# An attention scan and two expert layers on one core: the first chunk's scores in one readout, its y without a state, k turned on TensorE

## What is computed

```python
for t in range(S):                                   # S = 768, state 48 x 48 per head
    cur = einsum('bhd,bhe->bhde', u * kt, vt)
    y[:, :, t] = einsum('bhd,bhde->bhe', rt, state + cur)
    state = wt[..., None] * state + einsum('bhd,bhe->bhde', kt, vt)
x = y as 3072 tokens x 384
h = maximum(maximum(x @ w1, x @ w2), x @ w3); x = h @ w_out            # 384 -> 768 -> 384
h = x @ w_in; solu = h * softmax(h); out = layernorm(solu, g) @ w_out2  # 384 -> 1024 -> 384
```

## Time and profile before

| | us |
|---|---|
| median of 3 runs (lowest, highest) | 797.6 (792.9, 798.09) |
| the profiled execution | 798.28 |
| its span, first to last instruction | 796.4 |
| PE busy in the span | 744.8 (94%) |
| DVE busy | 502.3 (63%) |
| ACT busy | 296.6 (37%) |
| POOL busy | 70.6 (9%) |

### The profile page before, as it was taken

How to read it: one execution, slowest core, us unless ns; L and a number is a source line. 1 busy time by engine, 2 the same in 40 slices (tenths; PEclk the granted TensorE clock), 3 DMA queues, 4 the chain that set the end, 5 groups by cost and what they waited for, 6 DMA issues and landing times.

```text
span 796.4 us, 21297 instructions
## 1 busy us (share of the span) xinstructions
PE 744.8 (94%) x8960; PEld 619.4 (78%) x8960; DVE 502.3 (63%) x944; ACT 296.6 (37%) x698; POOL 70.6 (9%) x178
## 2 busy tenths in 40 slices
PE   4778799989999998999998999998999999999987
PEld 4667688868888877888876978877888877888766
DVE  5896764787556688465588655678654578322381
ACT  4344523555223346224245332246332336211261
POOL 2222211111011011010010110110110100000000
PEclk9965799989999999999999999999999999999999
DMA  6263630244411225501215502215611003400043
GB/s 240 74 196 122 189 107 24 68 134 155 129 54 38 63 78 181 163 22 56 76 43 181 190 12 76 77 32 152 206 35 59 2 9 114 142 11 0 1 140 112
DMA packets 56704, 74.89 MB, mean 94 GB/s; under 512 B 8224, under 2 KB 43296, under 8 KB 56608
## 3 DMA queue, kind: packets, MB, share of 16 engines
q1 hardware_dynamic: 56192, 73.44, 28.7%
q10 hardware_dynamic: 416, 0.08, 0.1%
HBM read 48.58 MB, written 22.54 MB: 89 GB/s over the span
## 4 chain that ended last, share of the span: by engine, by line
PE 80%; DVE 7%; SPq 5%; issue 3%; DMA 2%; ACT 2%; DVEq 0%; ACTq 0%
PE ps L666 17%; PE ps L607 16%; PE ps L609 14%; PE ps L608 14%; PE ps L564 11%; SPq L480 4%; PE ps L602 3%; PE ps L585 2%; PE ps L593 2%; DVE rk_sb L802 2%; DMA zT<-z_turning 1%; DVE scoresT L830 1%; SPq L472 1%; SPq L496 1%; DVE scoresT L823 1%
## 5 line engine op out<-in xcount | busy, mean ns | idle before, releaser
L666 PE MATMUL ps<-w_moe_out,zT 128*128 128x384 f32 x384 | 136.3, 509 | 10.0 <-DMA zT<-z_turning 6.2
L802 DVE TENSOR_TENSOR rk_sb<-rk_sb,decay 112x512 f32<-112x512 f32 x144 | 96.2, 689 | 65.2 <-PE ps L564 64.5
L666 PEld LDWEIGHTS ps<-w_moe_out,zT 128*128 128x128 f32 x384 | 118.8, 315 | 20.1 <-DMA zT<-z_turning 8.2
L607 PE MATMUL ps<-xT,w_moe 128*128 128x512 f32 x324 | 132.0, 408 | 0.0
L564 PEld LDWEIGHTS ps<-rk_sb 48*64 48x64 f32 x4224 | 86.9, 150 | 51.4 <-issue 37.2
L609 PE MATMUL ps<-xT,w_moe 128*128 128x512 f32 x324 | 126.8, 391 | 0.0
L608 PE MATMUL ps<-xT,w_moe 128*128 128x512 f32 x324 | 126.8, 391 | 0.0
L564 PE MATMUL ps<-rk_sb 48*64 48x32 f32 (+1 forms) x4224 | 98.5, 234 | 21.6 <-DVE rk_sb L802 18.7
L708 ACT COPY scoresT<-ps 16x128 f32<-16x128 f32 (+2 forms) x168 | 55.8, 332 | 103.0 <-PE ps L564 93.4
L830 DVE COPY_PREDICATED scoresT<-level_m,ps 64x256 f32<-64x256 uint32 x144 | 76.5, 532 | 2.8 <-issue 0.6
L751 ACT CAST h_x<-e_sb 128x512 fp32r<-128x512 f32 x36 | 22.3, 620 | 133.7 <-DVE e_sb L886 133.7
(11 more groups left out here) (78 smaller groups left out, 1001.4 us busy)
## 6 DMA issues: line engine op xcount, KB each, us to landing
rk_sb<-in_rk SPq DMA_DIRECT2D x24, 512.0 KB, 4.1
z_turning<-z_blocks SPq DMA_DIRECT2D x24, 512.0 KB, 3.1
zT<-z_turning SPq DMA_DIRECT2D x96, 128.0 KB, 2.8
w_sb<-in_w SPq DMA_DIRECT2D x24, 224.0 KB, 3.7
k_turning<-k_blocks SPq DMA_DIRECT2D x20, 256.0 KB, 2.2
k_tok<-k_turning SPq DMA_DIRECT2D x80, 64.0 KB, 2.2
v_sb<-in_v SPq DMA_DIRECT2D x24, 192.0 KB, 4.5
out<-out_sb SPq DMA_DIRECT2D x24, 192.0 KB, 2.1
```

The source lines that it names most:

```text
L607: nc.tensor.matmul(o, a[0], b[0], start=first, stop=False)
L666: last = nc.tensor.matmul(ps[:, OUT, 0:DM], zT[:, t % 2, :, c], w_moe2_out[:, c, :], start=(c == 0), stop=(c == J2 - 1))
L802: nc.vector.tensor_tensor(both, both, by, ALU.mult).then_inc(scaled, 1)
```

## The change

- **One readout for both halves** (groups 0 to 3, function `first`). DVE reads all 128 partitions in one instruction in slots 0 to 4. Both halves now go to the same 64 columns of `scoresT`; ACT's copies of levels 16 and 32 do too (`late %= HALF`). Partition rows of early tokens have their columns 64 to 127 for level 64 alone.
- **y of these groups** has no products with the state. It is formed in two halves by the scores' row (the token of k): rows 0 to 63 with all 128 columns, then, after a wait for the end of that (`y_early`), rows 64 to 127 with the last 64 columns. The last pair's v comes as a new input `v_pieces`, in pieces of 16 features behind 16 zeros, loaded into `z_blocks`; its y lands in the rows of `xT` that the repack filled, so these groups have no `y_last` and no repack. `u00` of the first chunk waits for `y_split` alone.
- **k of these groups** is turned by four PE transposes against an identity (a new input) into PSUM, and copied by ACT into `k_tok`. DVE's transposes, the two trips through DRAM and their waits go. ACT copies the update into the state (`turned`), since the state before it is zero.
- **All groups, level 2**: PE reads r's moving columns and DVE writes the result in the order (offset in the pair, pair), with the mask in that order too: DVE's inner run is 16 elements instead of 2.
- POOL clears the part of `scoresT` that later groups need zero after `M` of groups 2 and 3, and DVE's clear at the start goes.
- All four tables of the order are new.

```diff
+    . . u00 u01 . . u02 u10 . . u11 M v . . u12 u20 u21 . . d0 d1 u22 u30 u31 . . u32 d2 . y . u40 M v . . u41 u42 . .
...
 LAST = """
...
+        def v_piece(g, rows, k, i):
+            at = (i * KD + k) * V_PIECE
+            return v_first[rows, g, at:at + V_PIECE]
...
+        def first(g):
...
+            return g < FIRST_GROUPS
...
+            return (state_first, g + 1) if first(g) else (state_new, g - FIRST_GROUPS + 1)
...
         def y_of(g):
-            return y_aside[0:PR, :] if set_aside(g) else ps[0:PR, Y, :]
+            return y_aside[0:PR, :] if set_aside(g) else ps[0:C if first(g) else PR, Y, :]
...
             load_v(0)
+            sp.dma_start(v_first, v_pieces.rearrange("g p n -> p g n")).then_inc(v_first_loaded, 16)
             load_kr(2)
...
+                if first(g):
+                    return
...
+            def clear(g):
...
+                    pool.wait_ge(y_done, g + 1)
+                    nc.gpsimd.memset(scoresT[HB:128, g % RING_P, :, :, 0:HALF], 0.0).then_inc(cleared, 1)
...
                                 stationary, moving, width = k_sb[rows, slot, early], r_sb[rows, slot, q * C + HALF:(q + 1) * C], HALF
+                            if s == 2:
+                                moving = moving.rearrange("p n l -> p l n")
                             last = nc.tensor.matmul(ps[h * HALF:(h + 1) * HALF, banks[i], at + q * width:at + (q + 1) * width],
                                                     stationary, moving, start=True, stop=True)
...
+                    for q in range(PAIRS):
+                        for i, rows in enumerate((HB, D)):
+                            last = nc.tensor.matmul(upd[i * HB:i * HB + rows, q * D:(q + 1) * D], k_tok[:, i * HB:i * HB + rows, q],
+                                                    v_sb[:, (g - 1) % RING_K, (2 * q + i) * D:(2 * q + i + 1) * D], start=True, stop=True)
...
+                if g < PE_TURNED:
+                    if g == 0:
...
+                    else:
+                        pe.wait_ge(k_copied, g)
+                    for q in range(PAIRS):
+                        last = nc.tensor.transpose(ps[:, OUT, q * PR:(q + 1) * PR], k_sb[0:PR, slot, q * C:(q + 1) * C], ident[:])
+                    last.then_inc(k_on_rows, 1)
+                if first(g):
+                    update()
...
+                    for half in range(2):
+                        if half:
+                            pe.wait_ge(y_early, g + 1)
+                        rows, width = slice(half * HALF, (half + 1) * HALF), C - half * HALF
+                        for k in range(KD):
+                            for i in range(2):
+                                nc.tensor.matmul(yp[(i + 1) * HB - V_PIECE:(i + 1) * HB, k * C + half * HALF:(k + 1) * C], v_piece(g, rows, k, i),
+                                                 scoresT[rows, p, i, KD, 0:width], start=half == 0 and k == 0, stop=half == 1, skip_group_check=True)
+                        for q in range(KD):
+                            for i in range(2):
+                                last = nc.tensor.matmul(yp[i * HB:i * HB + D, q * C + half * HALF:(q + 1) * C], v_of(g, rows, q, i),
+                                                        scoresT[rows, p, i, q, 0:width], start=half == 0 and q == 0, stop=half == 1, skip_group_check=True)
+                        last.then_inc(y_done if half else y_early, 1)
...
+                wait_y()
+                signal, value = new_state_of(g - B)
+                pe.wait_ge(signal, value)
...
+                update()
+                wait_scores()
...
                 if n == 0:
                     wait_split(3 * KD)
-                    pe.wait_ge(repacked, B * REPACK * (m + 1))
                     if m:
+                        pe.wait_ge(repacked, REPACK * (B * (m + 1) - FIRST_GROUPS))
                         pe.wait_ge(var_done, 4 * m)
+                    else:
+                        pe.wait_ge(y_split, FIRST_GROUPS)
...
+                    if first(g) and L < HALF:
+                        late %= HALF
                     at = 0 if L == HALF else n * L % (HALF // 2)
                     last = nc.scalar.copy(dst[:, :, :, late:late + L], src[:, :, :, at:at + L])
...
+                if first(g):
+                    nc.scalar.copy(xT[:, 0, :, b * C:(b + 1) * C], y_tiles(g)).then_inc(y_hi, 1)
+                    return
...
+            def turned(g):
...
+                    act.wait_ge(group_done, g)
+                    nc.scalar.copy(state[0:PR, (g - 1) % B, :, 0:D], ps[0:PR, LEV[1], 0:PAIRS * D].rearrange("p (q d) -> p q d", q=PAIRS)).then_inc(state_first, 1)
+                if g < PE_TURNED:
+                    act.wait_ge(k_on_rows, g + 1)
+                    nc.scalar.copy(k_tok[:, 0:PR, :].rearrange("p f q -> p q f"),
+                                   ps[:, OUT, 0:PAIRS * PR].rearrange("p (q f) -> p q f", q=PAIRS)).then_inc(k_copied, 1)
...
-            nc.vector.memset(scoresT[HB:128, :, :, :, 0:HALF], 0.0).then_inc(cleared, 1)
-            dve.wait_ge(c_loaded, 16 * 2)
+            dve.wait_ge(c_loaded, 16 * 3)
...
+                for rows, at in ((slice(0, C), 0),) if first(g) else ((slice(0, HALF), 0), (slice(HALF, C), HALF)):
...
-                    dst = dst[:, :, :, h * HALF:(h + 1) * HALF]
+                    dst = dst[:, :, :, at:at + HALF]
...
-                        src = src.rearrange("p i q (n l) -> p i q n l", l=L)
-                        mk = level_m[rows, s - 2, :].rearrange("p (n l) -> p n l", l=L).unsqueeze(1).unsqueeze(1).to_broadcast([HALF, 2, PAIRS, HALF // 2 // L, L])
+                        if s == 2:
+
+                            outer, inner = inner, outer
+                            dst = dst.rearrange("p i q n l -> p i q l n")
+                        src = src.rearrange("p i q (a b) -> p i q a b", b=inner)
+                        mk = level_m[rows, s - 2, :].rearrange("p (a b) -> p a b", b=inner).unsqueeze(1).unsqueeze(1).to_broadcast([n, 2, PAIRS, outer, inner])
                         last = nc.vector.copy_predicated(dst, mk, src)
...
+                if first(g):
+                    x_hi, x_lo = (xT[:, p, :, b * C:(b + 1) * C] for p in range(2))
+                    nc.vector.tensor_tensor(x_lo, y_tiles(g), x_hi.bitcast(f32), ALU.subtract).then_inc(y_split, 1)
...
-                if not 0 <= g < UPDATED_GROUPS:
+                if not FIRST_GROUPS <= g < UPDATED_GROUPS:
...
-                if g < UPDATED_GROUPS:
+                if PE_TURNED <= g < UPDATED_GROUPS:
...
+    v_pieces = np.zeros((B, C, 2, KD, 2, PART), np.float32)
+    v_pieces[:, :, :, :, 1] = v[0:B, :, 2 * KD * D:].reshape(B, C, 2, KD, PART)
...
+        if i == 0:
+            late = late.reshape(-1, L).T.reshape(-1)
```

More of the change, by code:

```diff
@@ L509, in _, with clears_before @@
             nc.gpsimd.memset(state[:], 0.0).then_inc(cleared, 1)
+            def clears_before(kind, n):
+                here = PROGRAM.index((kind, (n,)))
+                return 1 + sum(kind == "M" and FIRST_GROUPS - RING_P <= task[0] < FIRST_GROUPS for kind, task in PROGRAM[:here])
             def tree(g):
```

144 lines of the change are left out of this document (89 added, 55 removed).

## The result

| | median us | lowest to highest | runs |
|---|---|---|---|
| before | 796.6 | 792.84 to 800.53 | 16 |
| changed | 800.14 | 797.76 to 803.11 | 16 |

Changed to before: 1.0049, 95% interval 1.0028 to 1.0069. The forecast was 782 with a range up to 797: it is wrong, on the wrong side of no change. The profiled execution of the changed kernel took 798.1 us, its span is 796.3 (before 796.4). So two spans of equal length are compared here, and the gain that was forecast has to be found where it was made and where it was given back.

A forecast was written before the change was run, and what follows sets the result against it. It took the start as a DVE-PE chain with DVE fuller, and PE's own work as the bound from 86.3 to 750 us. 798.3 less 11.3 in the start and 5 after gave 782 us, range 767 to 797.

The forecast's parts named there:

- Same products, same slots, so PE's 649 us stand: After the start, to 750 us: PE's busy time of 649 us would not change.
- Level 2 in the new order of its columns at the price of level 4: DVE's masked level 2: 0.44 us joined, like level 4; it might keep its 0.73 apiece, then 1.7 us less gain.
- Rival 1, strided columns slow PE: Level 2's slots, all 24 groups: PE reading columns 16 bytes apart costs 8 to 31 us, giving 790 to 813; chance 0.10.
- DVE in the start, 64.9 to 43.1 us: Up to the first expert product: joined readouts, k's turning and state work leaving DVE save 21.8 us of its busy time.
- Rival 4: DVE's joined readouts in the start cost what two did: 3.4 + 4.4 us return, 785 us; no chance of its own.
- PE in the start, 65.7 us: First four groups: transposes, y in two halves and a wait add 9.3 us to PE's 56.4 at the present clock.
- Idle time 24 to 6 us: PE's idle time in the start falls to about 6 us: 3 in the first slots, 6 x 0.4 at masked levels.
- The fuller PE should be granted 2.4 GHz more often: In the start: a higher PE clock brings the first expert product from 78 to 75 us, 3 us gained.
- rival 2: Clock stays at 1.2 GHz in the start, later order returns 0 to 2 us: 789 to 792 us; chance 0.20.
- rival 3: Clock opens to 2.4 GHz from about 40 us, first expert product at 62 to 66: 771 us; chance 0.22.
- After the start, 5 us: Behind the first expert product: 3.5 us from zT's DMA waits and 1.5 from ScalarE's squares; bounds 0 and 9.
- z's way back: zT's DMA at three chunk ends: issued 4 to 5 us earlier, it saves 3.5 of PE's 4.2 us of waits.

The follow-up runs named there:

- the version with both edits: The changed kernel with the identity allocated behind all other tensors and level 2 in its old order: 787.5 us, ratio 0.9889 to the kernel before.

## Why the prediction was wrong, step by step

- **"Same products, same slots, so PE's 649 us stand": the step that failed first.** Products and slots are the same, but a product is issued every 0.2324 us instead of every 0.2282. Between the places of the operands at a multiple of 256 bytes from each other and the others the medians differ by 5 to 6 us (786.5 to 787.5 against 792.1 to 793.1), by the pitch 7.3. That the diff adds a tensor in the middle of the allocation stood in front of me, and it had no term and no rival.
- **"Level 2 in the new order of its columns at the price of level 4", 0.44 us.** It costs 1.30. The range that I kept for it, 0.44 to 0.73, did not reach above what it had been, although my first rival was made of the same stride on the other engine. In medians it is 5.8 to 7.0 us of the result: about 2 of them in the start, the rest behind it, of which the wait at 151 us, with the low clock that follows it in some executions, is what I can show.
- **Rival 1, strided columns slow PE.** PE doesn't pay for them. The 64 score products with level 2's among them take 1.16 us at 85 us, against 1.14 at 92 us before. The mechanism existed one engine further, at DVE's write.
- **DVE in the start, 64.9 to 43.1 us.** 49.5, and 46.3 without the new order. Joined readouts at 0.42 to 0.43: right, and with level 2 as before they carry the gain, since splitting them costs 7.5 us. Rival 4 falls with it. But it was priced at 3 us, because DVE would be "no longer the bound", and that step is wrong: PE became the fuller engine, and the slots still wait for DVE's chain.
- **PE in the start, 65.7 us.** 63.7, and 64.3 in the version with both edits. Its parts, from the timeline of the changed kernel, group 0:

```profile
24.68 1.01 PE L657 MATMUL ps<-ident,rk_sb 112*128 112x112 f32 x4
25.62 1.49 PE L671 MATMUL ps<-scoresT,z_blocks 64*32 64x128 f32 x12
27.05 1.52 PE L675 MATMUL ps<-scoresT,v_sb 64*48 64x128 f32 x12
28.63 0.85 PE L671 MATMUL ps<-scoresT,z_blocks 64*32 64x64 f32 x12
```

  Four transposes in 0.94 us (1.7 forecast; the term has eight instructions where there are four). y's early half 3.0 (2.85), its late half from 28.63 to about 30.2, 1.6 (1.4), the wait between them not to be seen (0.25). Together 5.5 against 6.2.
- **Idle time 24 to 6 us.** 12.0 in the changed kernel, 9.2 in the version with both edits. PE still waits 6.8 us for the scaling, more than all the idle time of the forecast.
- **"The fuller PE should be granted 2.4 GHz more often", 3 us.** It was not. 32 score products take 1.08 us from 6 us up to the first expert product, which is the duration of 1.2 GHz, while the record says 1.00; before, they took 0.67 between 45 and 48 us. Only 2.7 us into the expert products, at 84.34 us, do these fall from 0.63 to 0.39. Here rival 2 was right and rival 3 wrong. The 0.73 that both the 3 us and rival 3 lean on the earlier trace rows is no better ground than the 1.00 at 36 us: it is a mean of 1.00 up to 47.7 us and 0.50 from there, and the first part is too high again. The 16 products with the state at 38.84 us take 1.96 us, as do those at 58.27 where the record says 0.50; only from 45.56 on are the durations short. The transposes, which by the Trainium skill ("TensorE: Matmul & The Clock Gate", Part 4) don't count as activity for the clock, aren't what keeps it low here: without them the start has the same durations. Why it stays low is open. With the 3 us taken back and the 3.2 us more of idle time, less the 1.4 us of PE, the sum gives 79.8; 79.5 were measured in the version with both edits (the 0.3 are the rounding of 77.7 to 78).
- **After the start, 5 us.** z's way back: right. PE's waits for it from 86 to 750 us fall from 4.2 to 0.2 us. ScalarE's squares: wrong, they stay (3.6 before).

```profile
PE ps L701 <- ACT ps L889: 3.5, 4, 1.0
...
PE ps L764 <- DMA zT<-z_turning: 0.2, 1, 0.2
```

  The stretch behind the first product is 714.6 us long, but 703.3 in the version with both edits against 710.1 before: 6.8 us won where 5 were forecast. Only part of that is the waits. Windows of before and of the version with both edits:

```profile
165.00:182.00 17.00, 14.32 (x137) 11.42 (x132) 14.00 (x29) 8.13 (x16) 0.00 (x0) 0.80 0.52 171
```

```profile
165.00:182.00 17.00, 14.98 (x216) 12.85 (x215) 14.28 (x30) 10.49 (x26) 0.00 (x0) 1.00 0.55 163
```

  Between the start and 750 us before's profiled execution has three stretches of 3.4 us at 0.50 (at 167, 177 and 430 us), the other none. The 72 expert products that span 154 to 213 us before take 3.4 us less in it. The forecast had this in its bound of 9 only, and it differs from one execution to the next: the changed kernel has one such stretch, at 173 us.

So only about half of what I forecast is there once the two costs are out. The profiled execution of the version with both edits, 784.57 us, comes within 2.6 of the 782, but it lies 2.9 below its median; by the medians and the ratio 0.9889 the gain is 8.8 us of 16.3. The start gives 6.8 of the 11.3, which leaves some 2 of the 5 for all that lies behind it (an estimate, a difference of medians and spans). Missing are the 3 us of clock, 3.2 us of idle time in the start and ScalarE's squares; for the rest no run names a cause. The changed kernel makes these gains too, and pays a little more for two things that were not meant to cost anything.

## What to carry to other kernels

A new tensor in SBUF can be a change to every instruction whose operands lie behind it, as it was to the 1728 products here. Put it last, or keep what stands behind it at its old remainder modulo 256 bytes, and when products whose code was not touched come at another pitch, look at the allocation first. When the order of elements is changed so that one side becomes contiguous, ask what becomes of the other side: price it from above as well, and measure the instruction alone before it goes into all groups. A start that is a chain between two engines pays nearly one for one for work on the engine that is waited for (7.8 us for some 9), also when the other engine is the fuller one.

## What the runs showed of the hardware that was not expected

- Matmuls of 512 fp32r columns with a stationary operand of 128x128 come every 0.2276 to 0.2281 us where moving and stationary tensor stand a multiple of 256 bytes from each other, whichever of the two places tried they have. From stationary to moving tensor, modulo 256, 64 bytes cost 0.0014 us a product (0.2293 to 0.2295), 128 bytes 0.0044 (0.2323 to 0.2325) and 192 bytes 0.0054 (0.2333 to 0.2334). The kernel before and eleven versions are of the first kind, the changed kernel and four versions of the others. The 64 were seen with moving weights alone and the 192 with moving activations alone. That loading weights and reading columns get in each other's way is the reading that fits; no run takes the two apart. The Trainium skill, in "SBUF — State Buffer", section "A bandwidth-pool intuition that's wrong (but worth ruling out)", gives the weight load a second, independent read port; by that the distance should not matter, and in these runs it does, by 0.6 to 2.4% of the pitch. Why 256 bytes is not shown.
- The last product (384 columns) takes 5.53 us for 16 matmuls in either case.
- A predicated copy by DVE of 256 values takes 0.42 us in runs of four or more, 0.73 in runs of two and 1.30 with single values every 16 bytes, on 64 and on 128 partitions alike.
- The granted clock in the record can be 1.00 over 75 us in which all durations are those of 1.2 GHz (32 score products 1.08 us, as at 63.00 us before, where it says 0.50); it is to be read with the duration of a known instruction beside it.
